# Four of the second mixer's weight units made during attention, the others spread over three supergroups

## What is computed

```python
q_s = softmax(q, axis=-1)      # per head, 8 heads of 64
k_s = softmax(k, axis=tokens)
x = q_s @ (k_s.T @ v)          # linear attention
u = x + (relu(x.T @ w_tok1) @ w_tok2).T      # token mixer, 576 -> 256 -> 576
y = u + relu(u @ w_ch1) @ w_ch2              # first channel mixer, 512 -> 1536 -> 512
xn = layernorm(y) * g
out = y + relu(xn @ v_ch1) @ v_ch2           # second channel mixer, 512 -> 2048 -> 512
```

## Time and profile before

| what | us |
|---|---|
| median of 3 runs | 1558.4 |
| lowest, highest | 1553.63, 1565.79 |
| the profiled execution | 1555.56 |
| its span | 1552.9 |

### The profile page before, as it was taken

The page is one execution under the profiler, slowest core; times in us unless marked ns, Lnnn a source line. Parts: engine busy times, 40 slices in busy tenths (PEclk is TensorE's granted clock), DMA queues, the critical chain, the costliest instruction groups (busy, mean ns, idle before and its releaser), DMA issues.

```text
span 1552.9 us, 19900 instructions
## 1 busy us (share of the span) xinstructions
PE 1482.3 (95%) x7656; PEld 1335.0 (86%) x7656; DVE 1054.0 (68%) x1177; ACT 685.8 (44%) x862; POOL 282.3 (18%) x299
## 2 busy tenths in 40 slices
PE   5999999997998999899989999999999999999998
PEld 5999998886787887788878888888888888889997
DVE  7889872583594594495695687568658856872276
ACT  5666552552452552453552453344345424532342
POOL 5445544662222213210000000000000000000000
PEclk9999999998999999999999999999999999999999
DMA  7787929769978979988758657776766686667765
GB/s 236 244 259 234 286 75 365 242 219 366 352 288 315 383 278 356 358 291 323 251 177 300 252 203 277 244 244 219 277 241 227 244 273 245 210 217 255 252 215 197
DMA packets 136605, 407.25 MB, mean 262 GB/s; under 512 B 13568, under 2 KB 34624, under 8 KB 136512
## 3 DMA queue, kind: packets, MB, share of 16 engines
q1 hardware_dynamic: 119040, 339.92, 62.9%
q0 software_dynamic: 17472, 66.07, 11.9%
HBM read 326.24 MB, written 79.69 MB: 261 GB/s over the span
## 4 chain that ended last, share of the span: by engine, by line
PE 73%; DMA 9%; DVE 8%; issue 5%; POOL 4%; ACT 1%; SPq 0%; POOLq 0%; DVEq 0%; ACTq 0%
PE ps L1325 23%; PE ps L1327 23%; PE ps L1326 23%; DMA w_ring<-w_scratch_B 5%; DMA w_op<-w1b 2%; DVE x_lo L953 1%; PE ps L1349 1%; DVE o_lo L1174 1%; DMA qt<-q 1%; DMA w_op<-w1c 1%; PE ps L1360 1%; PE ps L1440 1%; POOL w_op L485 1%; POOL w_op L483 1%; POOL w_op L487 1%
## 5 line engine op out<-in xcount | busy, mean ns | idle before, releaser
L1325 PE MATMUL ps<-x_hi,w_ring 128*128 128x462 f32 (+1 forms) x920 | 346.5, 377 | 29.7 <-issue 16.0
L1325 PE MATMUL ps<-o_hi,w_ring 128*128 128x462 f32 (+1 forms) x920 | 343.5, 373 | 13.1 <-DVE o_lo L1174 8.0
L1327 PE MATMUL ps<-x_hi,w_ring 128*128 128x462 f32 (+1 forms) x920 | 344.9, 375 | 0.0
L1326 PE MATMUL ps<-o_lo,w_ring 128*128 128x462 f32 (+1 forms) x920 | 341.6, 371 | 0.0
L1327 PE MATMUL ps<-o_hi,w_ring 128*128 128x462 f32 (+1 forms) x920 | 341.5, 371 | 0.0
L1326 PE MATMUL ps<-x_lo,w_ring 128*128 128x462 f32 (+1 forms) x896 | 335.7, 375 | 0.0
L793 ACT CAST o_hi<-h 128x924 fp32r<-128x924 f32 (+1 forms) x189 | 182.0, 963 | 229.7 <-PE ps L1327 206.5
L1174 DVE TENSOR_TENSOR o_lo<-h,o_hi 128x924 fp32r<-128x924 f32 (+1 forms) x189 | 214.6, 1138 | 58.4 <-ACT o_hi L793 58.4
L1325 PEld LDWEIGHTS ps<-x_hi,w_ring 128*128 128x128 f32 x920 | 175.3, 191 | 56.2 <-issue 30.8
L1325 PEld LDWEIGHTS ps<-o_hi,w_ring 128*128 128x128 f32 x920 | 173.1, 188 | 41.1 <-issue 15.7
L1144 DVE TENSOR_TENSOR h<-ps,h 128x924 f32<-128x924 f32 (+1 forms) x81 | 90.5, 1117 | 155.7 <-PE ps L1327 155.3
(11 more groups left out here) (165 smaller groups left out, 2147.5 us busy)
## 6 DMA issues: line engine op xcount, KB each, us to landing
w_ring<-w_scratch_C SPq DMA_DIRECT2D x280, 512.0 KB, 3.3
w_ring<-w_scratch_B SPq DMA_DIRECT2D x168, 512.0 KB, 5.0
w_scratch_C<-w_out POOLq DMA_DIRECT2D x16, 1792.0 KB, 12.4
w_scratch_B<-w_out POOLq DMA_DIRECT2D x12, 1792.0 KB, 8.2
kt<-kT SPq DMA_DIRECT2D x32, 288.0 KB, 5.7
u_scratch<-u_out SPq DMA_DIRECT2D x32, 288.0 KB, 2.8
qt<-q SPq DMA_DIRECT2D x32, 256.0 KB, 5.1
ke<-k SPq DMA_DIRECT2D x32, 256.0 KB, 5.1
```

The lines of the kernel that those rows point to most:

```text
L1325: mm(dst, a_hi, b_hi, start=start, stop=False, skip_group_check=onto)
L1326: mm(dst, a_hi, b_lo, start=False, stop=False, skip_group_check=onto)
L1327: return mm(dst, a_lo, b_hi, start=False, stop=stop, skip_group_check=onto)
```

## The change

Four of the 16 stage C units (n = 0 to 3 in the new count; `AHEAD` = 4) are made in the attention steps, with all work but the hi part on GpSimd: load of unit 0 in step 1, of 1 in step 3, of 2 in step 5, of 3 at the end of step 6; sums, hi, lo and store in steps 2, 4, 6 and 7. `lo_unit` is new on GpSimd. The stage B units are n = 4 to 15; n = 16 is made at the end of the plain product, 11 more by HI_AT, three in supergroup 1 and four in each of 2 and 3. For this the first stage B units move: loads of unit 4 at the end of step 6, of unit 5 in step 7; `hi_raw(0)` in step 7, `hi_raw(1)` in the plain product, `lo_raw(0)` at the end of step 7. `hi_px` and `lo_px` move back in step 7.

```diff
-    U0 = {"B": 0, "C": UNITS["B"]}
-    PLAIN = UNITS["B"]
-    HI_AT = {s * ENTRIES["B"] + e: PLAIN + 1 + 5 * s + i for s in range(3) for i, e in enumerate((0, 6, 11, 27, 36))}
+    AHEAD, PLAIN = 4, UNITS["B"]
+    ALL_UNITS = PLAIN + UNITS["C"]
+    HI_AT = {s * ENTRIES["B"] + e for s, at in enumerate(((5, 14, 25), (3, 11, 19, 27), (3, 11, 19, 27))) for e in at}
+    HI_AT = {e: AHEAD + PLAIN + 1 + i for i, e in enumerate(sorted(HI_AT))}
+    def unit_of(n):
+        if AHEAD <= n < AHEAD + PLAIN:
+            return "B", n - AHEAD
+        return "C", n if n < AHEAD else n - PLAIN
...
+            def lo_unit(n):
+                pool.wait_ge(wp_hi, n + 1)
+                for lo, hi in ((0, 4), (4, 7)):
+                    x = w_out[n % 2]
+                    nc.gpsimd.tensor_tensor(x[:, lo:hi, 1, :], w_op[:, n % 2, lo:hi, :], x[:, lo:hi, 0, :],
+                                            ALU.subtract).then_inc(wp_lo, 1)
...
@@ step of GpSimd
-                if i in (NB - 3, NB - 2):
-                    load_unit(i - (NB - 3))
+                if i % 2 == 1 and later:
+                    load_unit(i // 2)
                 if later:
                     sub_q(i + 1, ST)
+                if i % 2 == 0:
+                    sum_unit(i // 2 - 1)
+                if later:
                     lo_q(i + 1)
-                else:
-                    sum_unit(0)
-                    sum_unit(1)
+                if i % 2 == 0:
+                    lo_unit(i // 2 - 1)
+                    store_unit(i // 2 - 1)
+                if later == 1:
+                    load_unit(AHEAD - 1)
+                    load_unit(AHEAD)
+                if later == 0:
+                    sum_unit(AHEAD - 1)
+                    lo_unit(AHEAD - 1)
+                    store_unit(AHEAD - 1)
+                    load_unit(AHEAD + 1)
+                    sum_unit(AHEAD)
+                    sum_unit(AHEAD + 1)
...
@@ step of ScalarE
                     if later:
                         exp_k(i + 1, ST[0:1])
                     else:
-                        hi_px(0)
+                        hi_unit(AHEAD - 1)
                     hi_qT(i, ST[4:])
...
-                    hi_px(1)
+                    hi_px(0)
...
-                    if later == 0 and c < 2:
-                        hi_px(2 + c)
+                    if later == 0 and c < 3:
+                        hi_px(1 + c)
+                    if later == 0 and c == 2:
+                        hi_raw(0)
...
-                if later == 1:
-                    hi_raw(0)
-                    hi_raw(1)
+                if i % 2 == 0 and later and not first:
+                    hi_unit(i // 2 - 1)
...
@@ step of VectorE
-                if later == 0:
-                    lo_raw(1)
-                    lo_px(0)
-                    lo_px(1)
...
                     if later == 0 and c == 2:
-                        lo_px(2)
+                        lo_px(0)
+                        lo_px(1)
                 if later == 0:
+                    lo_px(2)
                     lo_px(3)
-                if later == 1:
                     lo_raw(0)
```

More of the change, by code:

```diff
@@ L396, in load_entry @@
                     units = 2 * c.j + 2 if c.j >= 0 else HC[c.stage] + 2 * e + 2
-                    units_stored(sp, U0[c.stage] + units)
+                    units_stored(sp, units + (AHEAD if c.stage == "B" else 0 if units <= AHEAD else PLAIN))
                 if n == RW - 1:
@@ L463, in load_unit @@
             def load_unit(n):
-                stage = "B" if n < U0["C"] else "C"
-                m = n - U0[stage]
+                stage, m = unit_of(n)
                 if m < HC[stage]:
@@ L552, in step @@
                     return
-                if i in (NB - 3, NB - 2):
-                    load_unit(i - (NB - 3))
+                if i % 2 == 1 and later:
+                    load_unit(i // 2)
                 if later:
                     sub_q(i + 1, ST)
+                if i % 2 == 0:
+                    sum_unit(i // 2 - 1)
+                if later:
                     lo_q(i + 1)
-                else:
-                    sum_unit(0)
-                    sum_unit(1)
+                if i % 2 == 0:
[11 more added lines that the diff above has]
+                    sum_unit(AHEAD + 1)
             batches(step)
-            for n in range(PLAIN):
-                if n >= 2:
+            for n in range(AHEAD, ALL_UNITS):
+                if n >= AHEAD + 2:
                     sum_unit(n)
-                store_unit(n)
-                load_unit(n + 2)
-            for n in range(PLAIN, U0["C"] + UNITS["C"]):
-                sum_unit(n)
-                if PLAIN + 2 <= n + 1 < U0["C"] + UNITS["C"]:
+                if n >= AHEAD + PLAIN and AHEAD + PLAIN + 2 <= n + 1 < ALL_UNITS:
                     load_unit(n + 1)
                 store_unit(n)
+                if n < AHEAD + PLAIN:
+                    load_unit(n + 2)
         @block.scalar
@@ L608, in hi_px, with hi_raw, hi_sums @@
                   .then_inc(px_hi_made, 1)
[L610 removed]
+            def hi_raw(p):
+                n = AHEAD + p
                 act.wait_ge(wp_in[n % 2], 32 * (n // 2 + 1))
                 wait(act, wp_stored[n % 2], 16 * (n // 2))
[L614 to L615 removed]
+                if p >= 2:
+                    act.wait_ge(groups, unit_over(p - 2))
                 x = w_op[:, n % 2, :, :]
                 nc.scalar.copy(w_out[n % 2][:, 0, 0, :], x[:, 0, :]).then_inc(raw_hi_made, 1)
[L618 removed]
+                nc.scalar.copy(plain_w(p, 0, 1)[:, 0, :], x[:, 7, :]).then_inc(raw_hi_made, 1)
                 nc.scalar.copy(w_out[n % 2][:, 5:7, 0, :], x[:, 5:7, :]).then_inc(raw_hi_made, 1)
[L621 removed]
+            def hi_sums(p):
+                n = AHEAD + p
                 act.wait_ge(wp_sum, 4 * (n + 1))
@@ L657, in plain @@
                 else:
-                    hi_unit(PLAIN)
+                    hi_unit(AHEAD + PLAIN)
                 if r < 2 * HC["B"]:
```

45 lines of the change are left out of this document (21 added, 24 removed).

## The result

The changed kernel takes 1576.3 us (median of 4 runs, 1574.4 to 1577.9), the kernel before in the same call 1558.9 (4 runs, 1553.6 to 1565.8). The ratio is 1.0114, 95% interval 1.0086 to 1.0142: 1.1% slower, where 0.8% faster was forecast, and above the range's end of 1563. The profiled execution took 1576.47 us over a span of 1574.7, so 21.8 us more span than before.

The account below looks back on a forecast made before the run. TensorE sets the pace in attention; stage B is bound by transfers, its 15 units the movable part. Terms +1.5 + 16.3 - 3.5 - 26 - 1 = -12.7 us give 1546 us against the median of 1558.4, range 1530 to 1563.

Parts of the forecast that it names:

- Part 1: Supergroups 1 to 3: four units fewer and wider spacing take off 9, 9 and 8 us, 26 in all (13 to 38).
- Part 2: Attention steps 2 to 6: GpSimd's sums beside norm_q cost 0.5 us for each of steps 3, 5 and 7, 1.5 (0 to 6).
- The transfers have room, but barely: Attention steps: 5.0 us of transfer time are free at a step's end, where a unit wants 5.9 to 7.0.
- rival (d): Steps 3 and 5 overrun through late kv_lo and delayed q, k and v loads, 19.8 us instead of 1: 1565 us; chance 0.11.
- Part 3: Step 7: TensorE waits 9.8 us behind unit 3's high part, slow clock 3, later tail 3.5: 16.3 us slower.
- Part 4: Plain product: one 1.8 MB store less stands before unit 2's load, 3.5 us off (0 to 4).
- The layer norm's wait: Before supergroup 4's layer norm: VectorE's 3.9 us wait for the last unit's store, counted as 1 us gained (0 to 3.9).
- (a): Supergroups 1 to 3: ring waits go almost wholly, gain 38 us instead of 26, 1534 us; chance 0.20.
- (c): Step 7: the load lands while ScalarE still waits for TensorE, saving 9.8 us but not the tail, 1536 us; chance 0.09.
- (b): Supergroups 1 to 3: ring waits half stay, blamed on x loads and y stores; gain 13 us, 1559 us; chance 0.14.
- signs of being wrong: Steps 3 and 5 over 27 us, supergroups at 107 to 110, or 2 and 3 over 112, or step 7 under 30.
- signs of being right: Step 7: TensorE idle 8 to 12 us, ScalarE waiting for sums, clock near half; supergroups 121, 110, 109; no VectorE w_scratch_C wait.

Follow-up runs that it names:

- e6: Kernel before with the second mixer's units 0 to 7 left out and the seven others all in supergroup 1: 1539.1 us, ratio 0.9897.
- e5: Kernel before with the second mixer's units 0 to 3 left out, the other eleven at old entries (0, 6, 11, 27): 1538.9 us, ratio 0.9890.
- e4: Kernel before with the second mixer's units 0 to 3 left out, the other eleven at the changed kernel's entries: 1551.4 us, ratio 0.9977.
- e1: Changed kernel with the stores of units 0 and 1 issued behind the q subtractions of steps 3 and 5, not at their heads: 1567.0 us, ratio 1.0075.
- e7: Changed kernel with three units ahead instead of four, late stores, and entries 0, 6, 11, 27 in supergroups 1 to 3: 1548.7 us, ratio 0.9950.
- e3: Changed kernel with entries 5, 11, 30 in supergroup 1 and 3, 9, 28, 36 in 2 and 3: 1570.7 us, ratio 1.0092.

## Why the prediction was wrong

The forecast was -12.7 us, the span showed +21.8: 34.5 us to account for.

- **"Part 1", four units fewer in supergroups 1 to 3: -26 forecast, -2.3 measured.** The largest error, and the step that turned the sign. That the units hold the supergroups was right (e6: 108.4 and 106.7 us without any). The size was taken as if bursts caused nearly all of it, so that one unit of five would bring 9 us of 11.5; by e5 it brings 3, and the whole term would be -14.8 (8.6, 3.0 and 3.2) at the old entries. That is near the lower bound of 13. The rest went to the new entries: 11.2 us between e5 and e4. I priced the moved entries by transfers only. What else a unit does at its entry, a high part on ScalarE, two lo parts on VectorE and four sums on GpSimd that hold VectorE up, was priced in the attention steps and left out in the supergroups, though rows 7 gave the size of the high part and the sums, and rows 10 what an overlap with GpSimd's work costs. TensorE's waits for o_lo in supergroups 2 and 3 rose from 0.4 to 10.4 us (13 stops in all three) while its waits for the ring there fell from 11.4 to 8.7 and "issue" from 6.2 to 0.3. So the ring, with the "issue" stops counted to it, did give back 8.6 us, and o_lo took 10.
- **"Part 2", steps 2 to 6: +1.5 forecast, +9.8 measured.** kv_lo was in time with no wait behind it, as worked out. The sentence "The transfers have room, but barely" was where it failed: it set 5.0 us free at a step's end against one unit's 5.9 to 7.0, and left the shortfall unpriced; and the store doesn't wait for the gap, it stands at the head of the step beside the v loads. That was rival (d), held at 0.11: its transfers' half came, with the mechanism that it named: steps 3 and 5 took 8.9 of its 19.8 us more, and e1 took 6.4 of them away. Its other half, kv_lo, did not come. Of the other 3.4 us of the 9.8 more than half is what the sums cost beside VectorE's norm_q, taken at 0.5 us a time: two norm_q took 2.73 us instead of 1.29 (below), so the lo parts of q, which wait for them, ended 3.28 us after the start of step 3 instead of 2.09. The 0.2 us that they had to spare were gone, and TensorE stopped for them in steps 3, 5 and 7:

```profile
105.72 0.39 PE L1408 MATMUL ps<-t_lo,q_hi 128*128 128x256 f32 x1 [0.73 <-POOL q_hi L533]
```

  That stop is there in every kernel with units ahead, and the head of steps 3 and 5 is 0.9 us longer in e1 and e7 too. The even steps cost 0.3 us each beside it, which no row singles out. By the rule of the Trainium skill, SBUF — State Buffer, "SBUF: two separate sides", the prediction worked out 1.5 us a step for the two norm_q. The trace agrees with 1.44, and TensorE followed 0.9 of it at the next step's head. VectorE's rows before and after, in an even step:

```profile
94.35 1.29 DVE L897 TENSOR_TENSOR qt<-qt,q_rec 128x512 f32<-128x512 f32 x2
```

```profile
93.78 2.73 DVE L925 TENSOR_TENSOR qt<-qt,q_rec 128x512 f32<-128x512 f32 x2
```

- **"Part 3", step 7: +16.3 forecast, +19.9 measured.** The chain was the one named, term by term: TensorE idle behind ScalarE's high part of unit 3, which waits for GpSimd's sums, which wait for the load. The load's rows:

```profile
223.36 0.72 POOL L485 DMA_DIRECT2D w_op<-w1c  x1
225.54 1.27 POOL L555 TENSOR_TENSOR kv_lo<-kv,kv_hi 128x512 fp32r<-128x512 f32 x1
231.78 0.72 POOL L491 TENSOR_TENSOR w_op<-w_op 128x256 f32<-128x256 f32 x1 [4.97 <-DMA w_op<-w1c]
```

  The load landed in 8.4 us, where 7.5 were taken. The wait was 13.29 us (9.8; range 6.5 to 13.5), the tail 5.71 (3.5; range 2 to 6), both near the end of what was allowed, and the granted clock behind the wait was 0.50 from 237 to 242 us. Of the 3.5 us that the wait was too long, 1.9 are the chain, which ended later after the start of the step than forecast, and 1.6 TensorE, which was ready earlier because a stop of 2.40 us before, behind the second transposes, was gone. The window rows close the sum: busy time rose by 2.9 us (20.95 to 23.83), the 3 us taken for the slow clock, and idle time by 17.0 (2.75 to 19.73: the two waits and the 0.73 us at the step's head).
- **"Part 4", the plain product: -3.5 forecast, -4.6 measured.** Right. The 2.91 us stop of the earlier trace rows is gone. In the bounds of the earlier trace rows, from which the forecast was made, 125.62 us became 122.4, so -3.3; the rest is the gap of 1.4 us in front of supergroup 1, which went.
- **The layer norm's wait: -1 forecast, -0.1 measured.** VectorE's 3.9 us for w_scratch_C went, as said, and the supergroup became no shorter: TensorE wasn't held by it.

Of the rivals, (a) and (c) fell. (b), ring waits that half stay, came nearest in size: it took 13 us for the four units, and e5 gave 14.8; but it blamed transfers for what stays, where the new entries' o_lo waits took most of it. Two of the signs of being wrong came, steps 3 and 5 over 27 us and supergroups 2 and 3 over 112. Of the signs of being right came ScalarE's wait for the sums in step 7, the clock of 0.50 behind it and VectorE's missing wait; TensorE's idle time was 13.3 us where 8 to 12 stood. The range of each term held for step 7 and the plain product; both terms that failed had their bounds drawn round a part of what happens in their place: in part 1 the transfers without the engines' work at the new entries, in part 2 the sums and kv_lo without the transfers.

Left open: supergroup 1 varies between 116.0 and 130.4 us over these kernels, with a stop of 2.9 to 7.3 us near its head in each, and which of its transfers decides that was not tried. How the rest of entry 19's cost divides between ScalarE's high part and VectorE's lo parts was not tried either. What causes the stops behind e3's entries 28 and 36 (1.09, 2.20 and 2.62 us in supergroup 2) was not taken apart.

## What to carry to other kernels

When background work is moved between the slots of a bound engine's schedule, price every engine that the work touches at its new slot, not only the resource whose crowding is the reason for the move: at a slot where VectorE runs without a pause, 2 us of its own work, 1.7 of ScalarE's and 3 of GpSimd's cost TensorE about 6 us of waits for it; at entry 11, with slack, they cost at most 0.3. Divide an excess by the number of items that cause it before you say what one is worth: the 11.5 and 9.3 us here over five units are 2.3 and 1.9 each, the runs gave 3.0 and 3.2, and the forecast took 9 and 8. And a large store is best issued behind the loads that the next step waits for: moving two of them past a few instructions took the ratio here from 1.0114 to 1.0075, some 6 us (the intervals overlap; the two steps in the traces give 6.4 us).
